# Seven products in place of eight for the first matmuls of two gated layers, run in three token thirds

## The reference

```python
scores = q @ k.T / 8 - slope * |distance|        # 4 batches, 8 heads, 576 positions, head size 64
attn   = softmax(scores, causal, window 128)
x = (attn @ v), heads side by side               # 2304 tokens x 512
x = (sigmoid(x @ w_gate) * (x @ w_val)) @ w_out  # 512 -> 1536 -> 512
y = ((x @ w1) * (x @ w2)) @ w3 @ w_out2          # 512 -> 1024 -> 1024 -> 512
```

## Time and profile before

| | |
|---|---|
| times of three executions | 968.31, 969.59 and 1548.55 us, median 969.59 |
| span of the profiled execution | 966.6 us |
| its own time | not listed apart; the two close times are 1.7 and 3.0 us above the span |
| PE busy | 937.0 us, 97% of the span, 4912 matmuls |
| DVE, ACT, POOL busy | 422.0, 315.3, 334.8 us |
| attention, up to the first layer matmul | 223.4 us |

### The profile page before, as it was taken

How to read it: one execution, slowest core, us unless ns; L and a number is a source line. 1 busy time by engine, 2 the same in 40 slices (tenths; PEclk the granted TensorE clock), 3 DMA queues, 4 the chain that set the end, 5 groups by cost and what they waited for, 6 DMA issues and landing times.

```text
span 966.6 us, 14591 instructions
## 1 busy us (share of the span) xinstructions
PE 937.0 (97%) x4912; PEld 799.1 (83%) x4912; DVE 422.0 (44%) x1115; ACT 315.3 (33%) x819; POOL 334.8 (35%) x314
## 2 busy tenths in 40 slices
PE   5899999999999999999999999999999999999998
PEld 4788888787888888888888888888888888888887
DVE  8999999994222222232232222345322222223223
ACT  6787888774211212121222121121121111121111
POOL 7677666661331231231231241231221222322211
DMA  6333333322010010010000000000000000000022
GB/s 217 104 114 108 96 109 102 106 101 77 22 44 1 22 44 1 22 43 0 22 24 19 22 22 22 22 22 22 22 22 22 22 22 22 1 0 1 1 87 109
DMA packets 28984, 44.95 MB, mean 47 GB/s; under 512 B 2464, under 2 KB 14368, under 8 KB 28960
## 3 DMA queue, kind: packets, MB, share of 16 engines
q1 hardware_dynamic: 28960, 44.64, 14.7%
HBM read 37.81 MB, written 6.82 MB: 46 GB/s over the span
## 4 chain that ended last, share of the span: by engine, by line
PE 80%; DVE 13%; issue 4%; ACT 1%; DMA 0%; SPq 0%; DVEq 0%; ACTq 0%
PE a_ps L374 9%; PE o_ps L375 9%; PE a_ps L375 9%; PE o_ps L374 9%; PE b_ps L375 8%; PE b_ps L374 8%; PE o_ps L376 8%; PE b_ps L376 8%; PE a_ps L376 8%; DVE pt_lo L691 3%; DVE rowsum L682 2%; DVE x_lo L699 2%; DVE w_hi L646 2%; DVE negs L671 2%; PE pv_ps L374 1%
## 5 line engine op out<-in xcount | busy, mean ns | idle before, releaser
L888 POOL TENSOR_TENSOR h_lo<-hid,h_hi 128x512 fp32r<-128x512 f32 (+1 forms) x100 | 118.0, 1180 | 555.9 <-ACT h_hi L607 555.9
L759 DVE TENSOR_TENSOR hid<-b_ps,side 128x512 f32<-128x512 f32 (+1 forms) x100 | 63.8, 638 | 406.2 <-PE b_ps L376 404.7
L604 ACT ACTIVATE side<-a_ps 128x512 f32<-128x512 f32 (+1 forms) x100 | 55.5, 555 | 483.2 <-PE a_ps L376 483.1
L374 PE MATMUL a_ps<-x_hi,w_hi 128*128 128x512 f32 (+1 forms) x400 | 147.4, 369 | 0.3 <-DVE w_lo L748 0.3
L375 PE MATMUL o_ps<-h_lo,w_hi 128*128 128x512 f32 (+1 forms) x400 | 147.3, 368 | 0.0
L375 PE MATMUL a_ps<-x_lo,w_hi 128*128 128x512 f32 (+1 forms) x400 | 147.3, 368 | 0.0
L374 PE MATMUL o_ps<-h_hi,w_hi 128*128 128x512 f32 (+1 forms) x400 | 147.3, 368 | 0.0
L375 PE MATMUL b_ps<-x_lo,w_hi 128*128 128x512 f32 (+1 forms) x400 | 147.2, 368 | 0.0
L376 PE MATMUL b_ps<-x_hi,w_lo 128*128 128x512 f32 (+1 forms) x400 | 147.2, 368 | 0.0
L376 PE MATMUL o_ps<-h_hi,w_lo 128*128 128x512 f32 (+1 forms) x400 | 147.2, 368 | 0.0
L376 PE MATMUL a_ps<-x_hi,w_lo 128*128 128x512 f32 (+1 forms) x400 | 147.2, 368 | 0.0
(11 more groups left out here) (69 smaller groups left out, 1440.9 us busy)
## 6 DMA issues: line engine op xcount, KB each, us to landing
k_raw<-kT SPq DMA_DIRECT2D x16, 288.0 KB, 2.8
q_raw<-qT SPq DMA_DIRECT2D x16, 288.0 KB, 2.8
v_raw<-v SPq DMA_DIRECT2D x16, 256.0 KB, 2.7
w_raw<-w3t SPq DMA_DIRECT2D x16, 256.0 KB, 3.1
w_raw<-w SPq DMA_DIRECT2D x8, 512.0 KB, 3.5
w_raw<-w_gate SPq DMA_DIRECT2D x6, 512.0 KB, 3.5
w_raw<-w_val SPq DMA_DIRECT2D x6, 512.0 KB, 3.5
w_raw<-w_out SPq DMA_DIRECT2D x6, 512.0 KB, 3.5
```

Source lines behind the costliest of these rows:

```text
L374: pe.matmul(out, lh, rh, start=start, stop=False)
L604: nc.scalar.activation(side[f][:, 0:n], ps_a[f][:, 0:n], func).then_inc(side_ready, 1)
L759: nc.vector.tensor_tensor(out=hid[f][:, 0:n], in0=ps_b[f][:, 0:n], in1=side[f][:, 0:n], op=ALU.mult).then_inc(hid_ready, 1)
L888: nc.gpsimd.tensor_tensor(out=h_lo[hb][f][:, 0:n], in0=hid[f][:, 0:n], in1=h_hi[hb][f][:, 0:n], op=ALU.subtract).then_inc(h_split, 1)
```

## The change

The program is almost wholly rewritten in its order, with these parts:

- **Strassen's recursion, one level, for `a` and `b`** (M1 to M7). The weight piece of a group (512 x 256) and the token block (512 x 768) are each seen as 2 x 2 blocks. Seven products of half size in each dimension take the place of eight. Sums and differences of weight blocks (`wsum`) and of token blocks (`xsum`) are made first, in fp32, and split into hi and lo; the seven results, in five PSUM banks, are combined by DVE and ACT.
- **Three passes.** The tokens are handled in three thirds of 768 (halves of 384 within each), each through both layers. A pass needs all ten groups, so 30 groups in all, and every weight is loaded, summed and split three times. Matmuls are 384 wide.
- The attention result is written once, in fp32, by ACT (`out_copy`); `x_hi` and `x_lo` of the attention are gone, and the fp32 sum also becomes the accumulator `xf`.
- Pairs are taken batch by batch; the bias is loaded once; the fold takes one product in each of 64 slots in a row; loops are gone, everything is written out.

The diff, cut to the parts that the steps below touch:

```diff
-x_hi = sb(ctx, "x_hi", [P, KB * T], F32R)
-x_lo = sb(ctx, "x_lo", [P, KB * T], F32R)
+xf = sb(ctx, "xf", [P, KB * T], F32)
+xs_hi = sb(ctx, "xs_hi", [P, 7 * 2 * TH], F32R)      # TH = 384
+xs_lo = sb(ctx, "xs_lo", [P, 7 * 2 * TH], F32R)
+BANK_OF = {M2: 0, M4: 1, M5: 2, M3: 3, M1: 4, M7: 1, M6: 4}
...
+def multiply(g, m, js):                               # PE; m = 0 for a, 1 for b
+    q, inst = 2 * g + m, instance(g)
+    if js[0] == M2:
+        pe.wait_ge(wq_split[m], g + 1)
+    for j in js:
+        if first_of(g) and m == 0:
+            pe.wait_ge(xs_split[j], inst + 1)
+        ...
+        elif j == M7:
+            pe.wait_ge(c_done[C21], q + 1)
+        elif j == M6:
+            pe.wait_ge(u11_done, q + 1)
+        for kk in range(2):
+            mm = product(quad_ps[BANK_OF[j]][:, 0:TH], ...)
+        mm.then_inc(prod_done, 1)
+def project(g):                                       # PE; 8 tiles on 3 banks
+    pe.wait_ge(wo_split, g + 1)
+    pe.wait_ge(h_split, 4 * (g + 1))
+    for k, (c, o) in enumerate(O_TILES):
+        t, hb = 8 * g + k, g % 2
+        wait(pe, acc_done, t - 2)
+        for f in range(FG):
+            mm = product(ps_o[t % 3][:, 0:TH], ...)
+for g in range(NG):                                   # PE, NG = 30
+    multiply(g, 0, ALL)
+    multiply(g, 1, ALL)
+    if not first_of(g):
+        project(g - 1)
+    if last_of(g):
+        project(g)
...
+def out_copy(n):                                      # ACT
+    for h in range(2):
+        op = nc.scalar.copy(out_cols(n, h), pv_cols(pC[n % 2], i, h))
+def weights_hi(g, m):                                 # ACT, 512 then 1280 elements
+    nc.scalar.copy(wq_hi[m][:, W_11 * GW:7 * GW]..., four[:, 0:4:3, :])
+    act.wait_ge(wsum_done[m], 3 * (g + 1))
+    nc.scalar.copy(wq_hi[m][:, 0:5 * GW], wsum[m][:, :])
+for g in range(NG):                                   # ACT
+    keep_21(2 * g)
+    out_hi(g)
+    keep_12(2 * g)
+    sigmoid(g, C21)
+    sigmoid(g, C12)
+    keep_21(2 * g + 1)
+    sigmoid(g, C11)
+    sigmoid(g, C22)
+    keep_12(2 * g + 1)
+    if more:
+        weights_hi(g + 1, 0)
+    for n, k in enumerate((C21, C12, C11, C22)):
+        hidden_hi(g, n, k)
+    if more:
+        weights_hi(g + 1, 1)
+        if last_of(g):
+            for j in (M2, M4, M5, M3, M1, M7, M6):
+                xs_hi_part(instance(g) + 1, j)
...
+def weight_sums(g, m):                                # DVE, inputs and output in SBUF
+    nc.vector.tensor_tensor(out=out[:, 0:2 * GW]..., in0=four[:, 0:4:2, :], in1=four[:, 1:4:2, :], op=ALU.add)
+    nc.vector.tensor_tensor(out=out[:, 2 * GW:4 * GW], in0=raw[:, 0:2 * GW], in1=raw[:, 2 * GW:4 * GW], ...)
+    nc.vector.tensor_tensor(out=out[:, 4 * GW:5 * GW], in0=raw[:, 0:GW], in1=raw[:, 3 * GW:4 * GW], op=ALU.add)
+def combine(g, m):                                    # DVE
+    dve.wait_ge(s21_done, q + 1)                      # s21: ACT's copy of M2 (keep_21)
+    C21 = M4 + s21
+    dve.wait_ge(s12_done, q + 1)                      # s12: ACT's copy of M5 (keep_12)
+    C12 = M3 + s12
+    t22 = M3 - s21
+    u11 = M1 - s12
+    if m == 1:
+        hidden(g, 0, C21)
+        hidden(g, 1, C12)
+    C11 = M7 + u11
+    C22 = M6 + t22
+    if m == 1:
+        hidden(g, 2, C11)
+        hidden(g, 3, C22)
+def hidden(g, n, k):                                  # DVE, inputs and output in SBUF
+    nc.vector.tensor_tensor(out=hid[:, piece(k)], in0=hid[:, piece(k)], in1=side[:, piece(k)], op=ALU.mult)
+for g in range(NG):                                   # DVE
+    combine(g, 0)
+    if more:
+        weight_sums(g + 1, 0)
+    combine(g, 1)
+    if not first_of(g):
+        add_up(g - 1)
+    if more:
+        weight_sums(g + 1, 1)
+    if last_of(g):
+        ...                                           # x_sum, x_lo_part and add_up(g) for the next instance
...
+for g in range(NG):                                   # POOL
+    out_lo(g)
+    if more:
+        weights_lo(g + 1, 0)                          # 512 then 1280 elements
+    for n, k in enumerate((C21, C12, C11, C22)):
+        hidden_lo(g, n, k)
+    if more:
+        weights_lo(g + 1, 1)
+        if last_of(g):
+            x_lo_part(inst, M5)
+            x_sum(inst, M7)
+            x_lo_part(inst, M7)
```

More of the change, by code:

```diff
@@ L43 @@
 IB = FF2 // P
-CH = 512
-CHUNKS = [slice(c, min(c + CH, T)) for c in range(0, T, CH)]
-NCH = len(CHUNKS)
 FG = 2
-G1, G2 = FF1 // (FG * P), FF2 // (FG * P)
-PIECE = KB * FG * P
+GW = FG * P
+PIECE = KB * GW
+G1, G2 = FF1 // GW, FF2 // GW
+GP = G1 + G2
+NPASS = 3
+TP = T // NPASS
+TH = TP // 2
+NG = NPASS * GP
+NQUAD = 2 * NG
 SCALE = 1.0 / D ** 0.5
@@ L115, in build @@
             v_lo = [sb(one, f"v_lo{b}", [P, VC * P], F32R) for b in range(2)]
-            bias = [sb(one, f"bias{b}", [P, KW], F32) for b in range(2)]
+            bias = sb(one, "bias", [P, HP * KW], F32)
             eye = sb(one, "eye", [P, P], F32)
@@ new lines, in build @@
+        h_lo = [sb(ctx, f"h_lo{b}", [P, 4 * TH], F32R) for b in range(2)]
+        s21 = sb(ctx, "s21", [P, TH], F32)
+        s12 = sb(ctx, "s12", [P, TH], F32)
+        u11 = sb(ctx, "u11", [P, TH], F32)
+        t22 = sb(ctx, "t22", [P, TH], F32)
+        xsum += [sb(ctx, f"xsum{k}", [P, 2 * TH], F32) for k in range(1, 5)]
+        qc, qd = [ctx.enter_context(nc.psum_tensor(f"quad_ps{k}", [P, 512], F32)) for k in (2, 3)]
+        qa, qb, qe = [ctx.enter_context(nc.psum_tensor(f"quad_ps{k}", [P, 512], F32)) for k in (0, 1, 4)]
@@ L369, in _, with product @@
+            last = NG - 1
+            store_half(last, 0)
+            for k in range(4, 8):
+                c, o = O_TILES[k]
+                sp.wait_ge(acc_done, after_tile(last, k))
+                tok = (last // GP) * TP + c * TH
+                sp.dma_start(out_v[:, o, tok:tok + TH], xf[:, acc_cols(last, c, o)]).then_inc(out_stored, 16)
+            sp.wait_ge(out_stored, 16 * (2 * (NPASS - 1) + 5))
         @block.tensor
         def _(pe):
-            def product(out, left, right, start=True, stop=True):
+            def product(out, left, right, start=True, stop=True, onto=False):
@@ L381, in scores @@
+                return pe.matmul(out, ll, rh, start=False, stop=stop, skip_group_check=onto)
+            def scores(n):
+                pair, i = where(n)
+                buf, pb = n % 2, pair % 2
                 if i == 0:
-                    pair = 2 * t + (s - LAG_QK) // STEPS
                     pe.wait_ge(k_split, pair + 1)
@@ new lines, in _ @@
+            ALL = (M2, M4, M5, M3, M1, M7, M6)
+            for s in range(SLOTS):
+                if s == NSTEP + LAG_TURN:
+                    multiply(0, 0, (M2, M4))
+                if 0 <= s - LAG_QK < NSTEP:
+                    scores(s - LAG_QK)
+                if 0 <= s - LAG_PV < NSTEP:
+                    pv(s - LAG_PV)
+                if 0 <= s - LAG_TURN < NSTEP:
+                    turn(s - LAG_TURN)
+                if 0 <= s - LAG_FOLD < NFOLD:
+                    fold(s - LAG_FOLD)
@@ L609, in group @@
-            def group(g, wb, func, more=True):
-                for c in range(NCH):
-                    chunk(g, c, wb, func)
-                    if more and 1 <= c <= 3:
-                        weights_hi(g + 1, c - 1, 1 - wb)
-            for s in range(LAG_OUT):
-                slot(ITERS, s)
-                if s == STEPS:
-                    act.wait_ge(fold_done, IB)
-                if STEPS <= s < STEPS + 3:
-                    weights_hi(0, s - STEPS, 0)
-            with act.Fori(0, G1 // 2) as gg:
-                for wb in range(2):
-                    group(2 * gg + wb, wb, ACT.Sigmoid)
@@ L624, in _ @@
-            for g in range(G1, G1 + G2):
-                group(g, g % 2, ACT.Copy, more=g + 1 < G1 + G2)
+                if XS_SLOT <= s < XS_SLOT + 7:
+                    xs_hi_part(0, s - XS_SLOT)
+                if s in (PREP_SLOT + 1, PREP_SLOT + 3):
+                    weights_hi(0, (s - PREP_SLOT) // 2)
+            for g in range(NG):
+                more = g + 1 < NG
+                keep_21(2 * g)
[16 more added lines that the diff above has]
+                            xs_hi_part(instance(g) + 1, j)
```

915 lines of the change are left out of this document (483 added, 432 removed).

## The result

| | before | after |
|---|---|---|
| device time, median of four runs each | 969.04 us | 1139.88 us (1137.49 to 1144.61) |
| ratio, with its 95% interval | | 1.177 (1.174 to 1.181) |
| span of the profiled execution | 966.6 us | 1135.7 us |
| first matmul of the layers | 223.4 us | 241.7 us |
| the layers, from there to the end | 743.2 us | 894.0 us |

One of the four executions of the kernel before took 1548.55 us, and the ratio is formed without it.

What follows compares the result with a forecast made beforehand. DVE was taken to bound the attention, PE's stream the layers. On the 966.6 us span, -52.8 stream, -8 attention and 181 us of stalls gave +120, so 1087; the median, 3.0 above, 1090 us, range 1000 to 1140.

Steps and rivals of the forecast that it cites:

- PE's stream: Layers' matmuls: 22.9 us a group, 686.4 us for thirty groups, a gain of 52.8 us.
- The exclusion: DVE instructions with two SBUF inputs and POOL ones reading SBUF take turns; `hidden` was to average near 1.4 us.
- The two waits of a middle group: PE waits 1.0 us for u11 before M6, and 2.8 us for a bank before the projection's fourth tile.
- the walk: One layer group followed engine by engine from PE's start at 0, ending at 26.7 us; extended to first groups and seams.
- the waits of the layers: PE's stalls in middle groups, first groups and seams, together 181 us, most of them put down to the exclusion.
- The seams: Layer one to two, three times 6.9 us; pass to pass, twice 11.5 us: 21 and 23 us lost.
- the sum: All gains and stalls against the 966.6 us span: +120 us; its first stall term was 24 x 1.0 + 6 x 6.2.
- The step: Attention estimate: 8 us better, bounds 15.8 better and 5 worse; `x_lo` removed, 12 us of DVE work added.
- Exclusion at no cost: Rival for the layers: DVE and POOL do not hold each other, 61 us of stalls, 970 us; chance 0.10.
- partly: Rival for the layers: slack missed by the walk leaves half the stalls, 1000 to 1045 us; chance 0.12.
- faster: Rival: order and exclusion both absorbed, only 17 us of seam stalls remain, 926 us; chance 0.06.
- the clock rival: PE slows after stalls: +21 us for the 11 longest, 1111; +46 for every projection wait, 1157, chance 0.04.

Runs made afterwards that it cites:

- experiment 4: Changed kernel with POOL's 1280-element subtraction of the first weight set replaced by three memsets that read nothing, low halves left out: 1045.48 us, ratio 1.080.
- experiment 9: experiment 6 with the first third's token sums and splits cut to one column per half block, first pass computing nothing of use: 1126.41 us.
- experiment 6: Changed kernel with SP issuing the layers' first two weight transfers in slot 61, at 155.2 us in place of 204.3: 1137.75 us, ratio 1.174.
- Experiment 5: Changed kernel with 24 unread 128-column matmuls ahead of the wait of the projection's fourth tile, except in each layer's last group: 1113.4 us, ratio 1.149.
- Experiments 6 and 7: experiment 6, and the changed kernel with the first third's token sums three slots apart from slot 48: 1138.04 us, ratio 1.175 for the latter.
- Experiment 10: Changed kernel with reordered POOL low halves and ACT copies, early first weight transfers, and DVE alternating sums and token operations between passes: 1014.38 us, ratio 1.047.

## Why the prediction was right in its mechanism and short in its size

**Right.** PE's stream, 132 x 0.1733 us a group: the pace is that to the last digit. The exclusion, by its price: a mean of 1.4 us for `hidden` was forecast, 1.420 is measured, with L860 and L824 at 0.55; experiment 4 shows that reading is what matters. The two waits of a middle group are where the walk put them, and a little shorter: from start to start M6 is late by 0.7 us (1.0 in the walk) and the fourth tile by 2.5 (2.8), and the groups without a slow stretch take 26.3 us (26.7).

POOL is busy in the layers for 493 us against 450; half of the difference is L1026, with 1188 ns where 1010 was forecast.

**Near by luck: the waits of the layers.** The walk gave them 181 us, the starts give 150 to 160. The seams, from the output-weight copy of a layer's last group to that of the next layer's third, hold 68.6 us of stream. With 1.0 twice, 6.2, 2.8 twice, 1.5 and the seam's 6.9 or 11.5 (the walk's 7.9 and 12.5 less the 1.0 that stands in the first term of the sum) the forecast was 90.8 us from layer one to two, and 95.4 from pass to pass. Measured are 92.6 to 95.2 and 98.8. That looks near, but it is made of waits of 18.2 to 18.5 us where 22.2 were forecast, and of 22.6 where 26.8 were, with 5.4 to 7.8 us of slow pace on top that the sum did not have.

**Wrong by 26 us: the attention**, forecast 8 us better, bounded at 5 us worse, measured 18.2 worse. The times of one and the same step show where. The reciprocal of step 56, of the kernel after:

```profile
156.25 0.17 DVE L743 RECIPROCAL recip<-rowsum 128x2 f32<-128x2 f32 x1
```

Before, the corresponding row of that kernel's trace is at 162.20. So up to the token work the new attention is 5.9 us ahead. The step put a gain there, for the removal of `x_lo` with its 43.6 us of DVE's work; which of the changes up to this point gave it was not taken apart. From there to the first product it is 61.2 us before and 85.4 after, 24.2 more. In this stretch DVE's busy time grows from 58.4 to 65.4 us only, and PE's clock, which was 1.00, is granted at 0.80 in the mean; columns as in the earlier trace rows, before and after:

```profile
162.20:223.40 61.20, 56.58 (x384) 49.20 (x382) 58.44 (x225) 49.22 (x169) 37.37 (x46) 1.00 0.30 97
156.30:241.60 85.30, 59.51 (x344) 52.96 (x343) 65.37 (x184) 56.15 (x176) 52.83 (x50) 0.80 0.21 65
```

The 24.2 us by the experiments:

- 12.9 us are the token work, with what it brings along of waits and slower clock (experiment 9 against 6). The step priced its nine operations at 0.95 each and put them into DVE's slack. But they come in pairs through two engines, DVE waits for ACT's rounding copy in between, and POOL holds some of them. One of the five subtractions and one of the four sums:

```profile
172.94 2.12 DVE L786 TENSOR_TENSOR xs_lo<-xsum,xs_hi 128x768 fp32r<-128x768 f32 x1 [2.24 <-ACT xs_hi L603]
...
176.39 1.87 DVE L777 TENSOR_TENSOR xsum<-xf 128x768 f32<-128x768 f32 x1
```

- 5.4 us are the wait for the first weights, which SP issued too late (experiment 6: 80.0 us left of 85.4). The step counted the weight sums but not the transfer ahead of them.
- 5.9 us are left in experiment 9 (67.05 against 61.2). They hold the weight sums with POOL's low halves, one of which holds a sum of DVE for 3.4 us, the fold products in every slot, and the slower clock, which is at 0.90 in this stretch of experiment 9 too. These were not told apart.

```profile
215.02 3.36 POOL L1014 TENSOR_TENSOR wq_lo<-wsum,wq_hi 128x1280 fp32r<-128x1280 f32 x1
...
215.54 3.39 DVE L799 TENSOR_TENSOR wsum<-raw_q 128x512 f32<-128x512 f32 x1
```

The failing was one of method: the exclusion had been found in the attention's own rows, and was then applied to the layers alone. Where work is added to DVE, with POOL at 139 of 200 us, the bound for "worse" had to hold it too.

**Wrong by 42 to 52 us, of which 23 show: PE's slower clock in the layers.** The sum put it at nothing. It was a rival, at 21 us for the longest stalls and at 67 us for every projection too, the latter with a chance of 0.04, and measured are 42 us (the starts at 0.32 alone) to 52. Since the waits came out 20 to 30 us shorter than the walk had them, the layers are only 22.6 us above the forecast (894.0 against 871.4). The argument was that gaps of 0.3 to 0.9 us had not brought the slow pace and only one of 2.32 us at the start had the earlier trace rows. But the rows just ahead of that wait show otherwise: before it PE's matmuls of 256 columns stand 0.21 us apart as well, from 8.67 to 9.95. So PE had been slow from its first matmul:

```profile
9.73 0.41 PE L375 MATMUL score_ps<-k_lo,q_hi 128*128 128x256 f32 x1
9.95 0.41 PE L376 MATMUL score_ps<-k_hi,q_lo 128*128 128x256 f32 x1
```

The longest gap of the kernel before in its full pace, 1.74 us ahead of 27.18, was followed by no slow matmul. No row of that kernel spoke for or against a gap of 2.8 us, the one that the walk put into every projection, so the zero in the sum and the 0.04 had no row behind them. It turned out in between: of twelve middle groups with the same 2.3 us gap, 8 have a slow stretch and 4 have none, at about 1.5 us each; the rest is in the seams and the groups behind them. Experiment 5, which leaves the waits and fills the gap in the projection, halves the slow pace, to 25 us. (The Trainium skill, TensorE: Matmul & The Clock Gate, "HAM oscillation", warns of idle gaps between bursts of matmuls; here the trace agrees, though not for each gap.) What decides in which group the clock falls stays open. Experiments 6 and 7 each started the layers some 4.5 us earlier, and their last output-weight copies are at 1104.69 and 1104.91, where the kernel after has it at 1104.44.

**The rivals.** Exclusion at no cost (970), partly (1000 to 1045) and faster (926) are out by the 1420 ns and the 67.3 us. The 1157 of the clock rival is above the measurement, since a third of the middle groups' gaps passed without it and the waits were shorter.

**Could the change pay?** Experiment 10 has 776.6 us of layers for the stream of 686.4, 90 us more; by the starts some 20 of these are still slow pace. Middle and second groups hold only 5 of these (23.3 and 22.6 us for a stream of 22.9). The six first groups hold 45, since they last 20.7 to 23.5 us for 14.6 of products, with no projection between them. The five seams hold 36 (37.9 and 39.1 for 31.2). Against the gain of 52.8 us stand these 81, and three passes make most of them, with six first groups and five seams. One pass would have two and one; it needs all tokens' seven blocks at once and was not tried. The attention ends 8 to 13 us later on top.

## What to carry to other kernels

A scheme that trades matmuls for additions moves work from a stream that has no waits to engines that share SBUF. Price each added operation of two SBUF inputs by what POOL reads at that moment, wherever in the program it stands, and ask for each large POOL operation which small DVE operation arrives in it: moving one call on POOL behind four small ones took off 85 us of 1140. Where a wait of PE cannot be taken away, price the clock that may fall after it as well, from the gap in the profile that is nearest to it in length, and look whether PE was at full pace ahead of that gap; where no such gap is there, the price belongs into the range. And compare a forecast with the measurement term by term: here waits that were 20 to 30 us too long hid half of a slow clock of 42 to 52.
